# Rescheduling a fused attention and channel-mixing kernel: first scaling on VectorE, batch steps in other slots, four splits moved to the next pair

## The chip, the cores and the metric

One core of a Trainium2 chip runs the whole program. The metric is the device time in microseconds (us) of one execution, as the median of several.

## The reference, cut to what matters

For 8 batches of 576 tokens, 8 heads of 64, the reference packs k and v through 32 pack rows p, attends from q to the packed rows, and feeds the result through two channel-mixing layers.

```python
def _attn_ref(q, k, v, p):
    p_packed = sm_attn(p, k, v)            # softmax(p k^T / 8) v
    out = sm_attn(q, p_packed, p_packed)   # 576 tokens against 32 packed rows
def _moe_ref(x, ...):                      # xk, xr: x mixed with the token before it
    k = np.maximum(xk @ w_k, 0.0)          # 512 -> 1024
    v = k * k @ w_v                        # 1024 -> 512
    r = 1.0 / (1.0 + np.exp(-(xr @ w_r)))
    return r * v
def _moe2_ref(x, U, V, w_ch1, w_ch2):
    u = x + (x.transpose(0, 2, 1) @ U @ V).transpose(0, 2, 1)
    return u + np.maximum(u @ w_ch1, 0.0) @ w_ch2   # 512 -> 2048 -> 512
```

All is float32. Large products are made from a high and a low part of each operand in three passes of TensorE. The last two products (w_ch1, w_ch2) are made with 7 block products instead of 8, from sums of blocks.

## The kernel before, in words

**One order for all engines.** `everything` (L1263) walks one list of items; each engine's block runs its own share of each item, in that order, and semaphores do the rest. An item's place is thus its place in all engines' queues at once. DMAs are issued by SP (HWDGE), by ScalarE in the first loads, and by GpSimd (the first p and v, the constants, the weights of the first layer, and the pieces).

**Start** (`first_items`, L179). Batch 0's attention runs alone, in the order of `UNIT_STEPS`: kA, kB (VectorE transposes k's four column blocks, L634/L636), p (GpSimd scales p by 1/8, L1477; VectorE transposes it, L648), scores1 (L532), a (L540), qA, pv (L552), pp (L558), qB, scores2 (L566), two softmax halves (sm, then norm0 and norm1, L677 to L688), outA and outB (L579). After scores2 and outB, TensorE makes 88 and 32 idle transposes (L1551). GpSimd issues p's four DMAs, v's ten, then scales p, then issues the constants (mu, U), then the weights' chunks, of which it also makes the low parts (L1507).

**Stage A** (`chunk_plan`, L121). Four groups of two batches (1152 tokens), each in 3 chunks of 384 tokens; the groups are called FIRST, MIDDLE (twice) and LAST. A chunk has 17 slots: 8 of k (12 matmuls of 384 columns, L780), 3 of r (12 of 512, L759), 6 of v (12 of 512, L794). Slots are counted through a group, 0 to 50. `batch_plans` (L98) puts the steps of the batches to come into slots: in group g a "second" batch (2g+1), a "third" (2g+2), and a "fourth" (2g+3), whose steps from slot 51 on fall into the next group ("rest"). A step is run behind the slot's own work. ("mix", "split") make a chunk's inputs from the attention's output x (L719, L732, L744, L751). `pe_g` (L863) reduces x2 with U. ScalarE and VectorE square k and split it (L814, L837, L803, L830).

**Pieces.** 32 pieces of w_ch1 and w_ch2 are loaded, combined by GpSimd (L1238 to L1243), split by ScalarE and VectorE (L1255, L1260) and stored in DRAM for stage B. The first `EARLY` of them use one buffer, during FIRST and MIDDLE, at the slots of `FIRST_AT` and `EARLY_AT`; the others (`piece_items`, L208) run in LAST with four buffers.

**Stage B** (`pair_plan`, L254). Five pairs of token tiles (512 wide three times, then 384), each with two groups g of hidden blocks; per g a first product m1 (4 units i of 7 positions, L1035) and a second m2 (28 entries e, L1121), each entry six matmuls with weights from `w_ring`, which SP loads 11 entries ahead (L1365). A pair's input u (L935, L940) is made during the pair before, its sums by GpSimd (L961 to L973), and its 14 combinations are split by ScalarE and VectorE (L994, L1000) as ("us", p, k). Position pos of m1 needs k = 2 pos and 2 pos + 1. In a pair's first unit `pe_m1` writes into banks that stage A has just used (`trio`, L456).

Of the kernel before, what the change touches and what calls it, by code (L numbers as in the profile page):

```python
# [34 lines left out]
VLOADS = 10  # L35
# [36 lines left out]
EARLY, FIRST_AT, EARLY_AT = 20, (22, 29, 36, 44), (0, 5, 10, 15, 23, 29, 35, 40)  # L72
# [25 lines left out]
def batch_plans(kind):  # L98


    third = (2, batch_slots(15, 17, 19, 20, 21, 22, 23, 25, 26, 28, 31, 33, 35))
    fourth = batch_slots(37, 39, 41, 42, 43, 44, 45, 47, 48, 50, 53, 55, 58)
    here = (3, {at: steps for at, steps in fourth.items() if at < CHUNKS * NSLOT})
    rest = (1, {at - CHUNKS * NSLOT: steps for at, steps in fourth.items() if at >= CHUNKS * NSLOT})
    if kind == FIRST:
        second = {2: ("scores1",), 4: ("a",), 5: ("qA",), 6: ("pv",), 7: ("qB", "pp"), 8: ("scores2",), 9: ("sm1",),
                  10: ("norm0",), 11: ("norm1",), 13: ("outA",), 14: ("outB",)}
        return [(1, second), third, here]
    return [rest, third, here] if kind == MIDDLE else [rest]
# [13 lines left out]
def chunk_plan(c, kind):  # L123
# [6 lines left out]
    for at, slot in enumerate(SLOTS):  # L130
# [32 lines left out]
        if kind == FIRST and c == 0 and at in (5, 6):  # L163
            items.append(("mix" if at == 5 else "split", 1, 0))
# [42 lines left out]
def piece_items():  # L207


    plan = {9: [("ws_load", EARLY + m) for m in range(SLOTS_P + 1)]}  # L210
    for m in range(PIECES - EARLY):
        n, at = EARLY + m, 12 + 8 * m // 5
# [36 lines left out]
U_SPOTS = [(0, 1), (0, 4), (1, 1), (1, 4), (2, 5), (3, 1), (3, 3), (3, 5)]  # L249
TURN_AT = (5, 11, 17, 23)  # L250


def pair_plan(p, left, turns):
# [3 lines left out]
    for g in range(NG):  # L257
        for i in range(NU):
            for pos in range(NPROD):
                items.append(("m1", g, i, pos))  # L260
                if p == 0 and g == 0 and i == 0 and pos < 5:
                    items += [[("x2s", 7, PAIRS - 1)], [("g", 7, 1, PAIRS - 1)], [("x2s", 8, PAIRS - 1)],
                              [("g", 8, 1, PAIRS - 1)], [("g_evac", 1, PAIRS - 1)]][pos]
# [19 lines left out]
        for e in range(NPROD * NU):  # L283
# [21 lines left out]
            if g == NG - 1 and p < NB - 1 and e % 2 == 1:  # L305
                items.append(("us", p + 1, e // 2))
# [28 lines left out]
class Attention:  # L335


    def __init__(self, sb, sem, scope):
# [22 lines left out]
        self.v_first_in, self.v_in = sem("v_first_in"), sem("v_in")  # L361
# [14 lines left out]
def build(nc, q, k, v, p, mu_k, mu_r, w_k, w_v, w_r, u, vv, w1, w2, out):  # L376
# [79 lines left out]
    trio = [{"X": (2, 4), "Y": (4, 2), "Z": (3, 3)}, {"X": (7, 5), "Y": (5, 7), "Z": (6, 6)}]  # L456
# [64 lines left out]
    def pe_attn(pe, n, step):  # L521
# [21 lines left out]
        elif step == "pv":  # L543
            if isinstance(n, int) and n == 0:
                pe.wait_ge(L.v_first_in, VLOADS * 16)
            else:
                pe.wait_ge(L.v_in, VLOADS * 16 * n)
# [92 lines left out]
    def dve_attn(dve, n, slot, step, mixes):  # L640
# [5 lines left out]
        elif step == "p":  # L646
            dve.wait_ge(L.p_scaled, n + 1)
# [355 lines left out]
    def pe_m1(pe, p, g, i, pos):  # L1003
# [7 lines left out]
        if pos in (R11, T1) and i < 2:  # L1011
# [3 lines left out]
            elif (pos, i) == (R11, 1):  # L1015
                pe.wait_ge(g_hi, B)
                pe.wait_ge(g_lo, B)
            elif (pos, i) == (T1, 1):
                pe.wait_ge(x2_ok, TPC * (NCH + 1))
# [722 lines left out]
```

## Time and profile before

| | us |
|---|---|
| median of 3 runs | 1409.76 |
| lowest, highest | 1403.69, 1412.27 |
| profiled execution | 1406.93 |
| its span, first to last instruction | 1405.1 |
| TensorE busy in the span | 1326.8 (94%) |
| VectorE, ScalarE, GpSimd busy | 912.5, 726.4, 222.5 |

TensorE is busy nearly all the time, so a time is read here as TensorE's work plus TensorE's idle stretches. Mean granted clock of TensorE is 0.988 of full. The start, up to TensorE's first matmul, takes 22.2 us; stage A ends at about 656 us; stage B and the last stores fill the rest.

### The profile page before, as it was taken

To read this page: it belongs to the slowest core of one execution; us is meant where nothing else is said; L and a number is where in the kernel's file an instruction comes from. 1 tells how busy PE (TensorE), PEld (TensorE's weight loads), DVE (VectorE), ACT (ScalarE), POOL (GpSimd) and SP (SyncE) were. 2 spreads that over 40 slices of the span, in tenths; PEclk is the share of its full clock that TensorE was granted. 3 is DMA by queue.
4 is the path that set the end of the run, shared out by engine and by line. 5 is a ranking of instruction groups with operands and counts; after the bars stand their busy time and mean duration, and the time that the engine had idled before them with its cause. 6 is when DMAs were issued, how large, how long until landed. Compare 5 with 4: busy or idle time off the path is not lost.

```text
span 1405.1 us, 21457 instructions
## 1 busy us (share of the span) xinstructions
PE 1326.8 (94%) x7712; PEld 1137.3 (81%) x7712; DVE 912.5 (65%) x1489; ACT 726.4 (52%) x1274; POOL 222.5 (16%) x306
## 2 busy tenths in 40 slices
PE   2889999999999999999999999999999999899997
PEld 1767787887888788987888788887888898899996
DVE  2777777677766876844563766549473776466746
ACT  1565664575557556644544645455453644365543
POOL 5830112212131103502000300012000200020000
PEclk9989999999999999999999999999999999999999
DMA  9653454555536512953756578765887578878986
GB/s 173 165 107 71 140 105 137 145 121 143 139 106 148 138 55 71 297 186 125 235 191 211 165 223 233 211 208 177 236 220 220 179 229 230 261 239 253 269 267 158
DMA packets 377001, 252.52 MB, mean 180 GB/s; under 512 B 249120, under 2 KB 291200, under 8 KB 376896
## 3 DMA queue, kind: packets, MB, share of 16 engines
q1 hardware_dynamic: 367136, 238.66, 60.3%
q0 software_dynamic: 5024, 11.90, 2.8%
q8 instruction: 62, 1.02, 0.3%
q10 hardware_dynamic: 4736, 0.59, 0.3%
q14 instruction: 43, 0.35, 0.1%
HBM read 201.25 MB, written 49.81 MB: 179 GB/s over the span
## 4 chain that ended last, share of the span: by engine, by line
PE 75%; DVE 10%; DMA 4%; issue 3%; ACT 3%; SPq 2%; POOL 2%; DVEq 0%; ACTq 0%; POOLq 0%
PE bank L1035 24%; PE bank L1121 21%; PE bank L780 9%; PE bank L794 9%; PE bank L759 6%; SPq L1295 2%; DMA w_ring<-w_parts 2%; PE bank L935 1%; DVE mixed L732 1%; DVE hid_parts L1150 1%; PE bank L863 1%; PE bank L579 1%; DVE acc L1169 1%; DMA early_raw<-in_moe_w_ch 1%; DVE u_parts L1000 1%
## 5 line engine op out<-in xcount | busy, mean ns | idle before, releaser
L1121 PE MATMUL bank<-hid_parts,w_ring 128*128 128x512 f32 (+1 forms) x1680 | 356.5, 370 | 10.0 <-DMA w_ring<-w_parts 4.7
L1035 PE MATMUL bank<-u_parts,w_ring 128*128 128x512 f32 (+1 forms) x1680 | 354.8, 369 | 2.8 <-ACT hid L1057 2.8
L1121 PEld LDWEIGHTS bank<-hid_parts,w_ring 128*128 128x128 f32 x1680 | 302.9, 188 | 62.1 <-issue 16.2
L1035 PEld LDWEIGHTS bank<-u_parts,w_ring 128*128 128x128 f32 x1680 | 306.2, 188 | 41.4 <-issue 3.1
L1144 ACT ACTIVATE hid_parts<-hid_raw 128x512 fp32r<-128x512 f32 (+1 forms) x280 | 164.8, 589 | 145.3 <-PE bank L1121 143.9
L1150 DVE TENSOR_TENSOR hid_parts<-hid_raw,hid_parts 128x512 fp32r<-128x512 f32 (+1 forms) x280 | 185.8, 669 | 67.0 <-ACT hid_parts L1144 63.4
L780 PE MATMUL bank<-xk_hi,wk_hi 128*128 128x384 f32 x384 | 132.1, 344 | 3.5 <-DVE xk_lo L751 3.5
L780 PE MATMUL bank<-xk_lo,wk_hi 128*128 128x384 f32 x384 | 130.0, 338 | 0.0
L780 PE MATMUL bank<-xk_hi,wk_lo 128*128 128x384 f32 x384 | 129.9, 338 | 0.0
L1080 DVE TENSOR_TENSOR hid_raw<-bank,hid_z 128x512 f32<-128x512 f32 (+1 forms) x40 | 25.5, 638 | 154.4 <-PE bank L1035 154.3
L794 PE MATMUL bank<-wv_hi,k_hi 128*128 128x512 f32 x288 | 113.4, 394 | 0.0
L794 PE MATMUL bank<-wv_lo,k_hi 128*128 128x512 f32 x288 | 112.2, 390 | 0.0
L794 PE MATMUL bank<-wv_hi,k_lo 128*128 128x512 f32 x288 | 112.1, 389 | 0.0
L814 ACT ACTIVATE square<-bank 128x384 f32<-128x384 f32 x96 | 47.0, 490 | 121.6 <-PE bank L780 101.3
L837 DVE TENSOR_TENSOR square<-square 128x384 f32<-128x384 f32 x96 | 57.3, 598 | 66.9 <-ACT square L814 66.5
L961 POOL TENSOR_TENSOR u_sums<-acc 128x512 f32<-128x512 f32 (+1 forms) x10 | 11.8, 1180 | 509.9 <-ACT acc L950 509.9
L780 PEld LDWEIGHTS bank<-xk_hi,wk_hi 128*128 128x128 f32 x384 | 73.3, 191 | 11.3 <-issue 8.6
L732 DVE SCALAR_TENSOR_TENSOR mixed<-x,mu,mixed 128x384 f32<-128x384 f32 x96 | 58.0, 666 | 32.1 <-ACT mixed L719 32.1
L1169 DVE TENSOR_TENSOR acc<-bank,acc 128x512 f32<-128x512 f32 (+1 forms) x120 | 73.9, 630 | 7.6 <-PE bank L1121 7.5
L780 PEld LDWEIGHTS bank<-xk_lo,wk_hi 128*128 128x128 f32 x384 | 73.3, 191 | 1.4
L780 PEld LDWEIGHTS bank<-xk_hi,wk_lo 128*128 128x128 f32 x384 | 73.1, 190 | 0.0
L794 PEld LDWEIGHTS bank<-wv_hi,k_hi 128*128 128x128 f32 x288 | 54.0, 188 | 13.8 <-issue 2.3
(156 smaller groups left out, 1934.5 us busy)
## 6 DMA issues: line engine op xcount, KB each, us to landing
w_ring<-w_parts SPq DMA_DIRECT2D x560, 256.0 KB, 3.5
w_parts<-early_out SPq DMA_DIRECT2D x23, 896.0 KB, 4.9
x_scratch<-x SPq DMA_DIRECT2D x36, 256.0 KB, 2.1
kq_parts<-in_k SPq DMA_DIRECT2D x120, 72.0 KB, 2.7
kq_parts<-in_q SPq DMA_DIRECT2D x112, 72.0 KB, 2.3
w_parts<-piece_out SPq DMA_DIRECT2D x9, 896.0 KB, 6.0
v_rows<-in_v SPq DMA_DIRECT2D x56, 128.0 KB
out_dram<-acc SPq DMA_DIRECT2D x84, 64.0 KB, 3.4
```

The lines of the kernel that those rows point to most:

```text
L732: last = nc.vector.scalar_tensor_tensor(out3, segments(c, ft, 0), mu[:, which, ft:ft + 1], out3, ALU.mult, ALU.add)
L759: last = nc.tensor.matmul(bank, a, b_, start=(done == 0), stop=(done == 3 * n_terms - 1))
L780: last = nc.tensor.matmul(bank[:, 0:CHUNK], wk[a][:, ct, at * P:(at + 1) * P], xk[b_][:, ct, :], start=(ct == 0 and a == 0 and b_ == 0), s ...
L794: last = nc.tensor.matmul(bank, k2[a][:, f, at * P:(at + 1) * P], wv[b_][:, f, :], start=(f == 0 and a == 0 and b_ == 0), stop=(f == NFA - ...
L814: nc.scalar.activation(square[:, at % 2, :], bank[:, 0:CHUNK], ACT.Relu).then_inc(k_ev, 1)
L837: nc.vector.tensor_tensor(square[:, at % 2, :], square[:, at % 2, :], square[:, at % 2, :], ALU.mult).then_inc(squared, 1)
L1035: last = nc.tensor.matmul(to, wring[:, e % RW, ct, a, :], uc[:, pos, b, ct, 0:w], start=(pos in FRESH and ct == 0 and a == 0 and b == 0), ...
L1121: last = nc.tensor.matmul(role(st, j, BANK_OF[pos])[:, 0:w], wring[:, e % RW, j, a, :], hid[:, no % RH, b, 0:w], start=(pos in FRESH and i ...
L1144: nc.scalar.activation(hid[:, no % RH, 0, 0:w], raw[:, pos, i, 0:w], ACT.Copy).then_inc(hid_hi, 1)
L1150: nc.vector.tensor_tensor(hid[:, no % RH, 1, 0:w], raw[:, pos, i, 0:w], hid[:, no % RH, 0, 0:w].bitcast(F32), ALU.subtract).then_inc(hid_l ...
L1169: nc.vector.tensor_tensor(to, role(st, j, name)[:, 0:w], to, ALU.add).then_inc(sum_ok, 1)
L1295: eng.dma_start(part[32 * quad:32 * quad + 32, :, :], src).then_inc(done, 16)
```

## The change

1. **First p and v.** VectorE waits for the first p's DMAs and scales it itself, in front of its transpose. GpSimd issues 6 of v's 10 first DMAs; ScalarE's queue issues the other 4, behind its part of k. TensorE's pv waits for both.
2. **Slots.** Steps of the third and fourth batch get other slots, in MIDDLE far earlier ones and more evenly spread (third from slot 6 instead of 15, fourth from 32 instead of 37). The second batch's steps move by up to one slot in FIRST; the first chunk's second mix and split move from slots 5 and 6 to 3 and 5.
3. **Pieces.** 18 instead of 20 run early, at other slots; the 14 of LAST begin three slots earlier.
4. **Stage B.** Per pair, 10 of the 14 splits stay in the m2 of the pair before, at 10 of its 28 entries; k = 10 to 13 move to the first four positions of the pair's own first unit. Before stage B's second unit, the last g work of stage A is spread over seven positions instead of five, with the banks of Z and X swapped on side 1 so that its bank is needed later.

```diff
-EARLY, FIRST_AT, EARLY_AT = 20, (22, 29, 36, 44), (0, 5, 10, 15, 23, 29, 35, 40)
+EARLY, FIRST_AT, EARLY_AT = 18, (23, 31, 38, 45), (0, 6, 11, 17, 23, 33, 40)
@@ batch_plans
-    third = (2, batch_slots(15, 17, 19, 20, 21, 22, 23, 25, 26, 28, 31, 33, 35))
-    fourth = batch_slots(37, 39, 41, 42, 43, 44, 45, 47, 48, 50, 53, 55, 58)
+    if kind == FIRST:
+        third = batch_slots(15, 17, 19, 20, 21, 22, 23, 25, 26, 28, 30, 34, 36)
+        fourth = batch_slots(37, 38, 40, 41, 42, 43, 44, 45, 47, 49, 50, 53, 55)
+    else:
+        third = batch_slots(6, 8, 11, 13, 15, 16, 17, 19, 21, 23, 25, 28, 30)
+        fourth = batch_slots(32, 33, 35, 37, 38, 39, 40, 42, 45, 47, 50, 53, 55)
-        second = {2: ("scores1",), 4: ("a",), 5: ("qA",), 6: ("pv",), 7: ("qB", "pp"), 8: ("scores2",), 9: ("sm1",),
-                  10: ("norm0",), 11: ("norm1",), 13: ("outA",), 14: ("outB",)}
+        second = {2: ("scores1",), 4: ("a",), 6: ("pv", "qA"), 7: ("qB",), 8: ("pp",), 9: ("scores2",),
+                  10: ("sm1", "norm0"), 11: ("norm1",), 13: ("outA",), 14: ("outB",)}
@@ chunk_plan
-        if kind == FIRST and c == 0 and at in (5, 6):
-            items.append(("mix" if at == 5 else "split", 1, 0))
+        if kind == FIRST and c == 0 and at in (3, 5):
+            items.append(("mix" if at == 3 else "split", 1, 0))
@@ piece_items
-    plan = {9: [("ws_load", EARLY + m) for m in range(SLOTS_P + 1)]}
+    plan = {6: [("ws_load", EARLY + m) for m in range(SLOTS_P + 1)]}
-        n, at = EARLY + m, 12 + 8 * m // 5
+        n, at = EARLY + m, 9 + 8 * m // 5
@@ pair_plan
+US_AT = (1, 4, 7, 9, 12, 15, 18, 20, 23, 25)
-                if p == 0 and g == 0 and i == 0 and pos < 5:
-                    items += [[("x2s", 7, PAIRS - 1)], [("g", 7, 1, PAIRS - 1)], [("x2s", 8, PAIRS - 1)],
-                              [("g", 8, 1, PAIRS - 1)], [("g_evac", 1, PAIRS - 1)]][pos]
+                if p == 0 and g == 0 and i == 0:
+                    items += {0: [("x2s", 7, PAIRS - 1)], 2: [("g", 7, 1, PAIRS - 1)], 3: [("x2s", 8, PAIRS - 1)],
+                              5: [("g", 8, 1, PAIRS - 1)], 6: [("g_evac", 1, PAIRS - 1)]}.get(pos, [])
+                if p > 0 and g == 0 and i == 0 and pos < 2 * NPROD - len(US_AT):
+                    items.append(("us", p, len(US_AT) + pos))
-            if g == NG - 1 and p < NB - 1 and e % 2 == 1:
-                items.append(("us", p + 1, e // 2))
+            if g == NG - 1 and p < NB - 1 and e in US_AT:
+                items.append(("us", p + 1, US_AT.index(e)))
@@ build
-    trio = [{"X": (2, 4), "Y": (4, 2), "Z": (3, 3)}, {"X": (7, 5), "Y": (5, 7), "Z": (6, 6)}]
+    trio = [{"X": (2, 4), "Y": (4, 2), "Z": (3, 3)}, {"X": (6, 5), "Y": (5, 6), "Z": (7, 7)}]
@@ pe_attn, dve_attn
-                pe.wait_ge(L.v_first_in, VLOADS * 16)
+                pe.wait_ge(L.v_first_in[0], 16 * 6)
+                pe.wait_ge(L.v_first_in[1], 16 * (VLOADS - 6))
+            if isinstance(n, int) and n == 0:
+                dve.wait_ge(L.p_first_in, 64)
+                nc.vector.tensor_scalar(L.pz[:, :, :], L.pz[:, :, :], SCALE, None, ALU.mult).then_inc(L.p_scaled, 1)
@@ pe_m1: the waits of (R11, unit 1) and (T1, unit 1) change places
@@ gpsimd
-        load_v(pool, 0)
-        scale_p(0)
+        load_v(pool, 0, range(6), att.v_first_in[0])
-                if k == 4:
+                if k == 2:
                     scale_p(2 * g + 3)
@@ scalar, start_loads
+                load_v(act, 0, range(6, VLOADS), att.v_first_in[1])
```

## Rows read from the trace of the kernel before

**Rows 1.** The page, parts 1 and 2: engines' busy time; granted clock in slices

```profile
PE 1326.8 (94%) x7712; PEld 1137.3 (81%) x7712; DVE 912.5 (65%) x1489; ACT 726.4 (52%) x1274; POOL 222.5 (16%) x306
PEclk9989999999999999999999999999999999999999
```

**Rows 2.** Waits of TensorE, 60 to 640 us: total us, times, longest

```profile
PE bank L579 <- DVE kqT L688: 10.7, 4, 3.1
PE bank L558 <- DVE packed L661: 4.9, 1, 4.9
PE bank L540 <- ACT probs L590: 1.6, 3, 0.8
PE bank L759 <- DVE xr_lo L751: 1.4, 1, 1.4
```

**Rows 3.** Timeline of the start: start, duration, engine, line [idle before]

```profile
5.36 4.79 POOL L1310 DMA_DIRECT2D v_rows<-in_v  x7
...
14.32 0.67 DVE L634 STREAM_TRANSPOSE kqT<-kq_parts 128x512 f32<-128x512 f32 x1
...
19.13 0.68 POOL L1310 DMA_DIRECT2D v_rows<-in_v  x1 [8.99 <-issue]
...
21.03 0.57 POOL L1477 TENSOR_SCALAR p_parts<-p_parts 128x128 f32<-128x128 f32 x1
...
21.64 0.31 DVE L648 STREAM_TRANSPOSE pT<-p_parts 128x128 f32<-128x128 f32 x1 [6.52 <-POOL p_parts L1477]
```

**Rows 4.** Tile views, p_parts then kq_parts_early, 0 to 60 us: DMA landing

```profile
DMA to landing us min/median/max: 2.7/3.0/3.5
DMA to landing us min/median/max: 2.9/6.1/10.4
```

**Rows 5.** Timeline, batch 0's last q blocks and what waits for them

```profile
6.55 18.30 SPq L1295 DMA_DIRECT2D kq_parts_early<-in_q  x16
...
30.85 1.43 DVE L638 STREAM_TRANSPOSE kqT<-kq_parts_early 128x576 f32<-128x576 f32 x2
...
32.43 1.20 PE L566 MATMUL bank<-kqT,packedT 64*32 64x288 f32 x32 [1.18 <-DVE kqT L638]
```

**Rows 6.** Windows: length, busy PE, PEld, DVE, ACT, POOL, PEclk, DMA share, GB/s

```profile
12.00:20.00 8.00, 0.00 (x0) 0.00 (x0) 2.27 (x6) 0.00 (x0) 0.87 (x2) 1.00 1.23 134
81.10:91.20 10.10, 6.46 (x29) 4.32 (x37) 7.81 (x15) 5.14 (x9) 3.42 (x6) 0.50 0.57 120
169.80:173.20 3.40, 3.40 (x24) 2.25 (x13) 2.71 (x4) 0.65 (x1) 1.03 (x3) 0.50 0.66 241
```

**Rows 7.** Timeline, the first chunk and the mix before it

```profile
49.93 5.17 DVE L732 SCALAR_TENSOR_TENSOR mixed<-x,mu,mixed 128x384 f32<-128x384 f32 x4 [1.39 <-ACT mixed L719]
...
79.60 2.19 DVE L732 SCALAR_TENSOR_TENSOR mixed<-x,mu,mixed 128x384 f32<-128x384 f32 x4
```

**Rows 8.** Lines of VectorE, 269.7 to 294.3 us

```profile
L830 DVE TENSOR_TENSOR k_lo<-square,k_hi 128x384 fp32r<-128x384 f32 x8 | 4.7, 583 | 0.0
```

**Rows 9.** Windows: a MIDDLE group's second chunk, its k slots

```profile
269.70:291.50 21.80, 21.80 (x225) 19.84 (x224) 15.60 (x31) 11.87 (x24) 4.72 (x8) 1.00 0.75 152
```

**Rows 10.** Waits of TensorE, 660 to 1165 us

```profile
PE bank L863 <- DVE x2s_lo L874: 1.6, 1, 1.6
```

**Rows 11.** Windows: end of the first pair, around entries 20 to 24

```profile
800.00:806.00 6.00, 5.37 (x22) 3.85 (x22) 6.00 (x9) 3.25 (x6) 2.48 (x2) 1.00 0.46 154
```

**Rows 12.** Waits of TensorE, 1165 to 1216 us

```profile
PE bank L1121 <- DMA w_ring<-w_parts: 4.7, 6, 1.8
PE bank L1035 <- ACT hid L1057: 2.8, 1, 2.8
```

**Rows 13.** Timeline of VectorE, one k_lo of the first chunk

```profile
71.85 1.09 DVE L830 TENSOR_TENSOR k_lo<-square,k_hi 128x384 fp32r<-128x384 f32 x1
```

**Rows 14.** Lines of VectorE, 309 to 320 us: two of norm0's and norm1's five operations

```profile
L688 DVE STREAM_TRANSPOSE kqT<-probs 128x576 f32<-128x576 f32 x2 | 1.6, 780 | 0.1
...
L677 DVE TENSOR_REDUCE tok_sum<-probs 128x18 f32<-128x576 f32 x2 | 1.5, 744 | 0.0
```

## What is predicted, and from what

> **What bounds the kernel now.** I read the page first: TensorE is busy 1326.8 of 1405.1 us and its clock is near full in every slice but the third [rows 1]. VectorE is far behind with 65%. So the change can win only TensorE's 78.3 us of idleness, and the half-clock stretches that follow some of it. Of the 78.3, 22.2 lie before the first matmul and the stores behind the last one also count; I looked for the rest in TensorE's waits. In stage A they are few and large: outA (L579) waits four times for the last transpose of a batch's normalised scores (10.7 us together, longest 3.1), pp waits once 4.9, the first r product once 1.4 [rows 2]. Stage B waits for little until 1165 us [rows 10, 11]; behind that lie 4.7 us for the weight ring and 2.8 for an evacuation held up by output stores [rows 12]. The last two are transfers' waits and no edit touches them; I count nothing there.
>
> The windows add the clock: 0.50 from 81.1 to 91.2 and from 169.8 to 173.2 [rows 6], and the same 3.4 us long from 320.0, where the third wait ends. Each begins during or right behind one of the waits of [rows 2] (1.2 for 2.4 GHz). At half clock the busy TensorE time does half its work: 6.46 / 2 = 3.2 us lost in the first, 3.4 / 2 = 1.7 in each of the others.
>
> **The start.** p's DMAs are issued in front of v's, which begin at 5.36 [rows 3], and land at most 3.5 us after their issue [rows 4], so p is there by about 9. GpSimd issues seven of v's DMAs, then stands 8.99 us, issues the rest and scales p at 21.03; VectorE, done with k at about 15.1, idles 6.52 us for it [rows 3]. After the change VectorE scales at 15.1. No row has this operation on VectorE; the bounds are 0.1 and GpSimd's 0.57, and I take the transpose of the same tile, 0.31. scores1 then starts near 15.9 instead of 22.2, 6.2 us earlier. What is late next is q: its last issue ends at 24.85, it lands 2.9 to 10.4 us after issue [rows 4, 5], and VectorE's last two q transposes took it without a wait at 30.85 [rows 5]. So it landed between 27.3 and 30.85; scores2 needs it plus 1.43 and ran at 32.43. With the middle, 29.1, scores2 comes at 30.7: gain 1.7. If only the second transpose is left after a landing at 27.3 it is 28.2, gain 4.2. On the other side, the weights' loads wait for VectorE's qA and now start some 5 us earlier, among q's last DMAs; a q that takes its longest landing, 10.4 after 24.4, gives scores2 at 36.3, a loss of 3.9. I take 1.7, range -3.9 to +4.2. Four DMAs on ScalarE's queue cost it nothing: its first work was the exponential behind scores1. Splitting v I count at nothing: the DMA share is 1.23 from 12 to 20 us [rows 6], so a second queue adds no transfer rate, and pv did not wait for v.
>
> The Trainium skill has the rule that speaks against this part (DMA: Bandwidth & Descriptors, "Issuing engines are not separate DMA queues": transfers from different engines share the same 16 DMA engines, a second issuer saves issue time only). By it the split of v brings 0; if a second queue were a second path, q would come early and the start would gain the whole 6.2. The share over 1 agrees with the rule.
>
> **The first chunk.** TensorE stands 4.9 us for pp, 1.4 for xr_lo, and loses 3.2 to the clock: 9.5 at stake. Now the mix comes two slots earlier and pp stands behind the first r. But a mix in slot 3 costs ScalarE 2.1 and VectorE 2.2 to 5.2 us in front of the copies that pv needs. Against TensorE's order, with 2.2, pv waits some 2 us and the first r starts at about 81 instead of 85.2; with 5.2 xr_lo is ready at 83. So 2.2 to 4.2 of the 6.3 idle, and the clock's 3.2 perhaps: range 2 to 9.5. I take 3.2 and half of the clock's, 4.8.
>
> The two prices of the mix are a row each: 5.17 us for four operations at 49.93, beside GpSimd's weight splits, and 2.19 at 79.60, when those end [rows 7]. The Trainium skill has a rule that speaks against this edit (SBUF — State Buffer, "Who interferes with whom": a VectorE instruction with two SBUF inputs contends with a GpSimd one that reads SBUF). Slot 3 lies among GpSimd's splits, so by the rule the edit brings 2.2, by the later row 4.2 plus the clock; the trace agrees with the rule at 49.93.
>
> **FIRST and MIDDLE.** In FIRST, outA waits 3.1 (slot 33) and 2.9 (slot 55), in each MIDDLE group once (slot 33; 2.2 and 2.7): the 10.7 of [rows 2]. All four have one cause: norm1, about 2.7 us of VectorE (five operations, three of some 0.75 [rows 14] and two small), stands two slots ahead of outA and behind a mix, a split or a piece. After the change the distance is four and three slots in FIRST, three in MIDDLE (8 us of TensorE). I count all 10.7, and the two clock stretches, 3.4: 14.1. Bounds: 0, if norm1 is late all the same, and 14.1. Steps that only spread cost no more work. In a MIDDLE group's second chunk the k slots get two softmax halves (three operations of 0.75 each) and norm0 (2.7), 7.2 us by the sizes of [rows 14], for transposes and maxima of about 6.9: VectorE goes from 15.6 of 21.8 [rows 9] to some 16 of about 19.3, since scores1, a and pv leave these slots. Busier, not full, but steps now arrive just in time at places where there was room. Such near misses are in the trace, L540's: three of 0.5 us [rows 2]. I take ten new ones at that price off, 5 us; bounds 0 and 10.
>
> **Pieces, loads.** Two pieces go from the early group to LAST, which starts three slots (7.6 us) earlier at the same rate; SP's loads wait only for batch 7's outB, now at slot 4 instead of 7. Cover: TensorE's own work in LAST, which had no idle stretch. Without cover one piece's 1.4 MB at 300 GB/s is 4.7 us, 9.4 in all. Scaling p for a fourth batch now stands in front of piece 3 instead of 5, long after its load. Nothing.
>
> **Stage B.** The g product in the first unit waits 1.6 us for VectorE, busy with splits [rows 10]; one position (1.37) later: 1.3, between 0 and 1.6. At the first pair's end VectorE is busy 6.00 of 6.00 us while TensorE idles 0.63 [rows 11]; four splits fewer are 4 x 0.68 = 2.7 us less of VectorE there. With the stretch before it and three more pairs' ends, 4 x 0.7 or 2.8 are at stake (an estimate from this one); I take 2.0, between 0 and 2.8. The four moved splits stand in front of left-over sums, 0.68 each, in a unit where VectorE has slack.
>
> **Sum.** 1.7 + 4.8 + 14.1 + 1.3 + 2.0 = 23.9, less 5: 18.9 us. Against the profiled span 1405.1 that is 1386.2. That execution took 1406.93; the median of the runs is 2.8 above it, so the median should go from 1409.8 to 1390.9.
>
> **Rivals.**
> - *The waits move along.* VectorE works in order; what was late at outA is late at pp, xr_lo or scores2. Then half of 23.9 comes and the 5 us of new waits stay: about 7, so 1403. For it: VectorE's share rises in the k slots. Against it: all four outA waits had one pattern.
> - *The first 90 us give nothing.* The weights' loads push q back (-3.9) and the first mix costs 5.2 (2.2): 18.9 - 5.6 - 2.6 = 10.7, so 1399. For it: the share over 1 [rows 6] and the 5.17 of [rows 7].
> - *Slower: VectorE overruns in the k slots.* If its 16 squares and low parts of a chunk run at 1.09 [rows 13] instead of 0.58 [rows 8] because of GpSimd, VectorE needs 16.0 + 16 x 0.51 = 24.2 for 19.3 us of TensorE: 4.9 lost in each of six chunks, 29, against 24 won and with the 5 of new waits: +10, so 1420. It decides once the mean passes 0.9. Against it: GpSimd is busy only 4.72 of 21.8 us there [rows 9], and has fewer pieces.
> - *Nothing happens.* It would need every moved step to be hidden; with waits of 22.2 and 10.7 that go by name I give it no chance of its own beside the first rival.
>
> **Chances.** The sum 0.62, on its own 1383 to 1396; waits moving along 0.25; first 90 us 0.08; slower 0.05. The range 1382 to 1403 takes in the first three down to the moving waits. A measurement tells about 1%, 14 us, from no change: below 1395.7 is faster. The forecast's case gives faster 0.62, the next two the same 0.33, the last slower 0.05.
>
> **What the profile would show.** scores1 at 16 and scores2 near 31; no wait over 1 us at L579 and L558; clock 1.00 at 170 and 320; first r near 82; g at stage B's start within 0.5 us; VectorE under 6 of 6 at the pairs' ends; and the waits of [rows 12] as they are. I am wrong if L558, L540 or L566 gather waits of 2 us in FIRST and MIDDLE, or if the stretch behind 1165 grows.

## The result, and the profile after

The changed kernel takes 1396.8 us (median of 6 executions, 1391.45 to 1400.04) against 1408.5 for the kernel before (6 executions beside it): ratio 0.9911, 95% interval 0.9882 to 0.9941. That is 12.5 us less (0.0089 x 1408.5). It lies inside the predicted range of 1382 to 1403 and 5.9 above the predicted 1390.9; it is just outside the 1383 to 1396 that the prediction gave its sum on its own, and above the 1395.7 below which it called the change faster. Three executions of kernels of the experiments (1486.5, 2671.7 and 3002.2 us) lie far above all others of the same kernel and are in no ratio. The profiled execution has a span of 1390.6 us, 14.5 less than before.

The page of the changed kernel, parts 1 and 2 (to be laid beside [rows 1]):

```profile
PE 1326.0 (95%) x7712; PEld 1136.3 (82%) x7712; DVE 912.7 (66%) x1490; ACT 717.4 (52%) x1268; POOL 214.1 (15%) x297
PEclk9899999999999999999999999999999999999998
```

TensorE's busy time hardly moves (1326.8 to 1326.0), as it should: its idle time falls from 78.3 to 64.6. Its waits from 60 to 640 us (engine, line and releaser: us in total, times, longest; L770, L547 and L874 are r, "a" and g), against [rows 2]:

```profile
PE bank L770 <- DVE xr_lo L762: 3.5, 1, 3.5
PE bank L770 <- ACT square L825: 2.2, 2, 1.8
PE bank L874 <- DVE x2s_lo L885: 1.9, 2, 1.4
PE bank L547 <- ACT probs L598: 1.3, 2, 0.7
PE bank L946 <- DVE v L1703: 1.2, 1, 1.2
```

All four outA waits (10.7 us in [rows 2]) are gone, and so is pp's of 4.9. The first r's wait for xr_lo grew from 1.4 to 3.5. r's wait for ScalarE's square is new, and g's for x2s_lo grew from 0.5 (before's row below) to 1.9.

```profile
PE bank L863 <- DVE x2s_lo L874: 0.5, 1, 0.5
```

Timeline of the start (start, duration, engine, line, in brackets the idle time before and its releaser), against [rows 3, 5]:

```profile
14.85 0.71 DVE L642 STREAM_TRANSPOSE kqT<-kq_parts 128x512 f32<-128x512 f32 x1 [7.37 <-DMA kq_parts<-in_k]
...
17.05 0.19 DVE L657 TENSOR_SCALAR p_parts<-p_parts 128x128 f32<-128x128 f32 x1
...
17.84 2.17 PE L539 MATMUL bank<-kqT,pT 64*32 64x288 f32 x32 [17.84 <-DVE pT L659]
...
25.99 1.60 POOL L1501 DMA_DIRECT2D stage_r<-in_moe_w_k  x3 [3.16 <-DVE kqT L646]
...
26.32 0.33 PE L566 MATMUL bank<-ident,packed 128*128 128x128 f32 x1 [0.57 <-DVE packed L672]
...
31.32 0.78 DVE L646 STREAM_TRANSPOSE kqT<-kq_parts_early 128x576 f32<-128x576 f32 x1 [3.12 <-DMA kq_parts_early<-in_q]
...
32.24 2.18 PE L574 MATMUL bank<-kqT,packedT 64*32 64x288 f32 x32 [5.59 <-DVE kqT L646]
```

scores1 comes 4.4 us earlier, pp 4.6, and scores2 0.2: a wait of 5.6 us for q has taken nearly the whole gain. Windows of the changed kernel (length, busy PE, PEld, DVE, ACT, POOL, PEclk, DMA share, GB/s): the start, the first r, the places of the two half-clock stretches of [rows 6], and the first pair's end [rows 11]:

```profile
28.00:38.30 10.30, 6.06 (x51) 4.72 (x52) 4.66 (x7) 1.39 (x2) 0.82 (x2) 0.50 0.97 291
82.60:89.50 6.90, 5.87 (x14) 4.57 (x15) 6.80 (x14) 3.09 (x5) 1.75 (x3) 0.51 0.43 132
168.50:172.00 3.50, 3.50 (x22) 3.50 (x22) 3.50 (x7) 1.61 (x4) 1.44 (x2) 1.00 0.55 182
317.00:321.00 4.00, 4.00 (x49) 3.11 (x48) 4.00 (x7) 2.82 (x5) 1.76 (x3) 1.00 0.89 150
787.50:793.50 6.00, 5.91 (x26) 4.28 (x25) 5.95 (x9) 3.08 (x6) 1.77 (x2) 1.00 0.56 168
```

The two stretches in stage A are at 1.00. The one of the first chunk is 6.9 us long instead of 10.1, and there is a new one of 10.3 us at the start, where before ran at full clock:

```profile
28.00:38.30 10.30, 8.63 (x159) 7.39 (x158) 6.14 (x11) 2.83 (x5) 2.84 (x6) 1.00 1.00 302
```

Added up from the first matmul to 1300 us, the profile before has 27.3 us at half clock and the changed one has 27.3 as well: what stage A won back, the start took.

Stage B's waits, against [rows 10, 12] (L1046 is m1, L1132 m2):

```profile
PE bank L1046 <- DVE hid_raw L1091: 0.9, 1, 0.9
...
PE bank L1132 <- DMA w_ring<-w_parts: 3.2, 4, 1.1
PE bank L1046 <- ACT hid L1068: 2.4, 1, 2.4
```

To see where time comes from, take the moment at which TensorE starts a stage and compare it with the same moment in the profile of before. In us, negative is earlier (the kernels of the last columns follow below):

| TensorE starts | before at | changed | without part 1 | slots alone | chunk alone | part 4 alone | start alone |
|---|---|---|---|---|---|---|---|
| scores2, batch 0 | 32.43 | -0.2 | +0.5 | -0.2 | -1.0 | +0.5 | +6.4 |
| first k | 56.12 | +0.7 | +0.5 | -0.7 | -1.0 | -0.2 | +6.7 |
| first r | 85.21 | -1.6 | -2.1 | 0.0 | -3.6 | +0.3 | +7.8 |
| k, FIRST's second chunk | 116.19 | -1.5 | -2.4 | -1.2 | -4.0 | -0.8 | +6.6 |
| k, second MIDDLE, first chunk | 372.94 | -10.6 | -10.9 | -11.8 | -2.4 | -1.9 | +4.2 |
| k, LAST's first chunk | 518.99 | -11.7 | -11.9 | -15.3 | +1.5 | -1.9 | +5.5 |
| stage B | 656.7 | -12.2 | -13.5 | -17.2 | -0.3 | -3.7 | +3.7 |
| second pair's m1 | 821.45 | -13.4 | -14.6 | -17.2 | -0.4 | -4.9 | +3.7 |
| third pair's m1 | 983.03 | -14.3 | -15.6 | -17.2 | -0.4 | -5.8 | +3.7 |
| fifth pair's m1 | 1276.46 | -15.6 | -17.2 | -13.9 | +1.4 | -5.8 | +1.6 |

One profile is one execution, and executions of one kernel lie up to 9 us apart (23 of the kernel before run from 1401.7 to 1410.7); a column shows where steps come, not their size to the microsecond.

### The profile page after: what moved, and what is told of

Read it like the earlier page. It is cut to its first block, busy times and chain, and to the rows that moved or that the text cites. A ratio compares the mean times of both kernels' runs of the same rounds, so it can differ in the third digit from the quotient of the medians.

```text
span 1390.6 us, 21451 instructions
## 1 busy us (share of the span) xinstructions
PE 1326.0 (95%) x7712; PEld 1136.3 (82%) x7712; DVE 912.7 (66%) x1490; ACT 717.4 (52%) x1268; POOL 214.1 (15%) x297
## 4 chain that ended last, share of the span: by engine, by line
PE 76%; DVE 9%; SPq 6%; DMA 4%; issue 2%; ACT 2%; POOL 0%; DVEq 0%; ACTq 0%
PE bank L1046 25%; PE bank L1132 23%; PE bank L805 9%; PE bank L791 8%; PE bank L770 6%; SPq L1306 3%; DVE mixed L743 2%; DMA w_ring<-w_parts 1%; PE bank L946 1%; SPq L1321 1%; DMA w_parts<-early_out 1%; PE bank L1559 1%; PE bank L874 1%; PE bank L587 1%; DVE square L848 1%
## 5 line engine op out<-in xcount | busy, mean ns | idle before, releaser
L1132 PE MATMUL bank<-hid_parts,w_ring 128*128 128x512 f32 (+1 forms) x1680 | 356.4, 370 | 6.6 <-DMA w_ring<-w_parts 3.2
L1046 PE MATMUL bank<-u_parts,w_ring 128*128 128x512 f32 (+1 forms) x1680 | 355.4, 369 | 3.8 <-ACT hid L1068 2.4
L1132 PEld LDWEIGHTS bank<-hid_parts,w_ring 128*128 128x128 f32 x1680 | 302.9, 188 | 58.5 <-issue 14.1
L1046 PEld LDWEIGHTS bank<-u_parts,w_ring 128*128 128x128 f32 x1680 | 305.8, 188 | 43.5 <-issue 4.4
L972 POOL TENSOR_TENSOR u_sums<-acc 128x512 f32<-128x512 f32 (+1 forms) x10 | 11.7, 1179 | 493.4 <-ACT acc L961 493.4
L791 PEld LDWEIGHTS bank<-xk_hi,wk_hi 128*128 128x128 f32 x384 | 72.9, 190 | 14.9 <-issue 9.4
L743 DVE SCALAR_TENSOR_TENSOR mixed<-x,mu,mixed 128x384 f32<-128x384 f32 x96 | 59.9, 684 | 29.1 <-ACT mixed L730 28.8
L805 PEld LDWEIGHTS bank<-wv_hi,k_hi 128*128 128x128 f32 x288 | 54.0, 188 | 15.9 <-issue 4.0
```

The lines of the kernel that those rows point to most:

```text
L743: last = nc.vector.scalar_tensor_tensor(out3, segments(c, ft, 0), mu[:, which, ft:ft + 1], out3, ALU.mult, ALU.add)
L791: last = nc.tensor.matmul(bank[:, 0:CHUNK], wk[a][:, ct, at * P:(at + 1) * P], xk[b_][:, ct, :], start=(ct == 0 and a == 0 and b_ == 0), s ...
L805: last = nc.tensor.matmul(bank, k2[a][:, f, at * P:(at + 1) * P], wv[b_][:, f, :], start=(f == 0 and a == 0 and b_ == 0), stop=(f == NFA - ...
L1046: last = nc.tensor.matmul(to, wring[:, e % RW, ct, a, :], uc[:, pos, b, ct, 0:w], start=(pos in FRESH and ct == 0 and a == 0 and b == 0), ...
L1132: last = nc.tensor.matmul(role(st, j, BANK_OF[pos])[:, 0:w], wring[:, e % RW, j, a, :], hid[:, no % RH, b, 0:w], start=(pos in FRESH and i ...
```

## Experiments: each part alone

**Part 1 alone** (the first p and v as in the changed kernel, all else as before):

```
+            if isinstance(n, int) and n == 0:
+                dve.wait_ge(L.p_first_in, 64)
+                nc.vector.tensor_scalar(L.pz[:, :, :], L.pz[:, :, :], SCALE, None, ALU.mult)...
-        load_v(pool, 0)
-        scale_p(0)
+        load_v(pool, 0, range(6), att.v_first_in[0])
+                load_v(act, 0, range(6, VLOADS), att.v_first_in[1])
```

> The kernel before with part 1 of the change alone (VectorE scales the first p, v over two queues). Two theories. Clock theory: q still lands last, near 31, so scores2 stays at 32.2; TensorE idles 5.6 us in front of it and drops to half clock there, so the 88 idle transposes end late, outA comes at about 46.0 instead of 44.9, the first k group at 56.8 instead of 56.1 and batch 1's scores1 at 65.7 instead of 64.1: +1.5 us in all, ratio 1.000 to 1.002. Rival, as the prediction had it: the 4.4 us that scores1 gains are partly kept, first k group at 54.4 or sooner and 1.7 us off the total, ratio 0.9988.

1410.1 us against 1406.3, ratio 1.0027 [1.0008, 1.0047], 12 executions: 3.8 us slower. Its timeline:

```profile
37.85 0.78 DVE L639 STREAM_TRANSPOSE kqT<-kq_parts_early 128x576 f32<-128x576 f32 x1 [8.89 <-DMA kq_parts_early<-in_q]
...
38.78 2.18 PE L567 MATMUL bank<-kqT,packedT 64*32 64x288 f32 x32 [12.18 <-DVE kqT L639]
```

The last block of q is there at 37.8, beyond even the prediction's worst case (a scores2 at 36.3). Of the two theories on record neither had this; the one that expected a loss had q near 31 and 1.5 us.

**The changed kernel without part 1** (the lines above undone).

> The changed kernel without part 1. Clock theory: the first r group comes at 82.0 instead of 83.6 and everything behind it 1.6 us earlier, total 1395.2 against 1396.8, ratio 0.990. Rival (the start did help): first k group as before at 56.1 but total 1 to 4 us above the changed kernel, ratio 0.992 to 0.994.

1388.9 us, 0.9878 [0.9858, 0.9898]. That is 4.6 us better than the changed kernel (0.0033 of 1406), and its 4 executions lie within 4.3 us, the changed kernel's within 8.6. Both numbers that were expected (0.990, or 0.992 to 0.994) were too high. The two intervals overlap a little (0.9882 to 0.9898), so the size is uncertain, but with everything else in place part 1 seems to cost as much as alone. Its profile has 17.1 us at half clock up to 1300 us, where the changed kernel's has 27.3.

**Third and fourth batch's slots alone.** `EARLY`, the pieces' slots, the second batch and stage B are as before; the MIDDLE groups' lines of the edit:

```
-    third = (2, batch_slots(15, 17, 19, 20, 21, 22, 23, 25, 26, 28, 31, 33, 35))
-    fourth = batch_slots(37, 39, 41, 42, 43, 44, 45, 47, 48, 50, 53, 55, 58)
+        third = batch_slots(6, 8, 11, 13, 15, 16, 17, 19, 21, 23, 25, 28, 30)
+        fourth = batch_slots(32, 33, 35, 37, 38, 39, 40, 42, 45, 47, 50, 53, 55)
```

> The kernel before with the third and fourth batches' slots alone (pieces, first chunk, start and stage B as before). If the waits of outA are removed by the slots themselves: no wait over 1 us at L579 behind 100 us, full clock at 170 and 320 us, and about 10 us off (4.9 in FIRST, 5.3 in MIDDLE as the changed kernel shows them), ratio 0.993. Rival: the slots need the new places of the pieces (18 instead of 20 early ones, six slots apart) and without them ScalarE or VectorE holds up the k groups; then 3 to 6 us off, ratio 0.996 to 0.998.

1392.9 us, 0.9905 [0.9887, 0.9922]: 13.4 us, where about 10 was expected; the rival, that the slots need the pieces' new places, fell. The table's column goes from -1.2 to -15.3 by LAST: 14.1. Its waits from 60 to 640 us still have those of the first chunk, and at outA's matmuls none for kqT (one of 0.4 for x):

```profile
PE bank L562 <- DVE packed L665: 4.5, 1, 4.5
PE bank L536 <- DVE pT L652: 2.0, 2, 1.1
PE bank L763 <- DVE xr_lo L755: 1.4, 1, 1.4
```

**Part 4 alone.** In short:

```
+US_AT = (1, 4, 7, 9, 12, 15, 18, 20, 23, 25)
-            if g == NG - 1 and p < NB - 1 and e % 2 == 1:
+            if g == NG - 1 and p < NB - 1 and e in US_AT:
```

> The kernel before with part 4 alone (four splits into the next pair, g work spread, banks swapped). From the changed kernel's trace: 0.2 us at stage B's start, 1.0 us at the end of each of pairs 1, 2 and 4, and at most 0.9 in the ring's waits behind 1165 us: 3.4 off, less 1.1 that the last stores took back, ratio 0.998. Rival: the gain of pairs 3 and 4 in the changed kernel was the DMA's chance and not the splits'; then only the first two pairs' ends gain, 2.0, ratio 0.9985, and the waits for the ring stay at 4.7.

1403.7 us, 0.9983 [0.9969, 0.9997]: 2.4 us. The column's -3.7 at the start of stage B is no effect of it, as stage A is that of before: 1.8 of it is u's wait of 1.7 at 619 us, which before's profile has and this one hasn't. Its own are the two steps of 1.0 at the first and second pair's ends.

**The first chunk alone** (with the second batch's slots):

```
-        if kind == FIRST and c == 0 and at in (5, 6):
+        if kind == FIRST and c == 0 and at in (3, 5):
```

> The kernel before with the first chunk's edit alone: the second batch's steps in their new slots of FIRST, and the first chunk's second mix and split in slots 3 and 5. Theory: what the whole changed kernel gained between the first k and the first r product (2.3 us; 2.6 without part 1) belongs to this edit alone, and the next outA too: first r 2.5 us earlier than before, the end 2.5 to 5 us earlier, ratio about 0.9975. Rival: the edit gains nothing alone (the waits at L579 behind it are met again later): ratio 1.000. By the prediction's term of 4.8 it would be 0.9966.

1401.7 us, 0.998 [0.9966, 0.9994]: 2.8 us. First r is 3.6 earlier, 2.6 of it behind the first k. In this profile the gain is lost again, and the waits from 60 to 640 us and the windows say how:

```profile
PE bank L579 <- DVE kqT L688: 12.2, 4, 4.1
PE bank L759 <- DVE xr_lo L751: 4.0, 1, 4.0
```

```profile
233.00:237.00 4.00, 4.00 (x15) 3.65 (x15) 2.23 (x4) 1.94 (x5) 2.10 (x4) 0.57 0.05 19
465.50:472.30 6.80, 5.50 (x29) 4.33 (x30) 4.19 (x6) 0.65 (x1) 1.74 (x4) 0.50 0.58 196
```

The same places in the kernel before:

```profile
233.00:237.00 4.00, 1.11 (x19) 0.36 (x18) 3.86 (x8) 1.42 (x3) 1.20 (x2) 1.00 0.82 260
466.00:470.00 4.00, 2.19 (x24) 1.61 (x25) 3.93 (x7) 0.65 (x1) 0.00 (x0) 1.00 0.93 309
```

In this execution two of the four outA waits became longer (3.2 for 2.9 and 4.1 for 2.7), and the clock fell behind both, which before's profile passed at full clock. But it took 1408.4 and is the slowest of its twelve: by time, over all twelve, the 2.8 us do arrive.

## Experiments: why the start costs

**Weights' loads held back.** The changed kernel, with the loads of the first layer's weights waiting for all eight transposes of k and q.

```
-        pool.wait_ge(att.kq_ok, CT + 2)
+        pool.wait_ge(att.kq_ok, KQ)
```

> The changed kernel, but GpSimd starts the weights' loads only when all of batch 0's q is transposed (a wait for 8 instead of 6). Rival theory (the weights' 2.6 MB among q's last DMAs push q back): q lands near 29, scores2 at 30 or below, first k group not before 55.5, total 3 to 5 us below the changed kernel, 1392 to 1394. If v's second queue is what counts: q lands near 30.5 to 31, scores2 at 31.5 to 32, and the weights, 4 us later, hold up the first k group or the first v group instead; total the same or 1 to 3 us more, 1397 to 1400.

1388.5 us, 0.9887 [0.9867, 0.9906]; timeline:

```profile
29.43 0.78 DVE L646 STREAM_TRANSPOSE kqT<-kq_parts_early 128x576 f32<-128x576 f32 x1 [1.30 <-DMA kq_parts_early<-in_q]
30.36 2.17 PE L574 MATMUL bank<-kqT,packedT 64*32 64x288 f32 x32 [4.29 <-DVE kqT L646]
30.51 1.60 POOL L1501 DMA_DIRECT2D stage_r<-in_moe_w_k  x3 [7.11 <-DVE kqT L646]
```

The weights start at 30.5 instead of 26.0, q is in at 29.4 instead of 31.3, scores2 gains 2.1 over before, and weights that come later held nothing up: the first k is 1.7 and the first r 4.0 us earlier than before. The time came out 4 us better than the 1392 to 1394 expected, though the ratio's interval and the changed kernel's still overlap (0.9882 to 0.9906).

**The same edit on part 1 alone.**

> The kernel before with part 1 of the change alone, and GpSimd's loads of the first weights waiting until VectorE has transposed all eight column blocks of q and k (instead of the first six). Theory: part 1 by itself cost 6.4 us at scores2 because the weights' loads, asked for 5 us earlier, ran among q's last DMAs; with the wait q is in by about 29.5, scores2 comes near 30.4 to 30.9 (32.43 before), the first r product not later than before, and the ratio is at or below 1.000 (about -1.5 us, 0.999). Rival: it is v's split over two queues that pushes q back (k's last block already landed 2 us later with it); then q still lands behind 31, scores2 comes at 33 or later and the ratio stays near 1.0027. Second rival: weights that come late hold up the first chunk by 2 us or more, then scores2 is early and the first k product is not.

```profile
29.08 0.78 DVE L639 STREAM_TRANSPOSE kqT<-kq_parts_early 128x576 f32<-128x576 f32 x1 [0.82 <-DMA kq_parts_early<-in_q]
...
30.01 2.18 PE L567 MATMUL bank<-kqT,packedT 64*32 64x288 f32 x32 [3.36 <-DVE kqT L639]
```

q is in at 29.1 instead of 37.8, with v still on two queues. All six profiles that have part 1 with the split agree: with the weights' loads beside, q's last block is in at 31.2, 31.3 and 37.8, with the weights held back at 28.8, 29.1 and 29.4. So the weights' loads are needed for the delay. Whether they are enough is for the next experiment. First r is 1.9 earlier than before, FIRST's last r 3.4. By time it is 1.0009 [0.9993, 1.0025]: no longer a loss that shows, but no gain either (and the interval overlaps that of part 1 alone). In its profile 3.4 at 193 us is 1.5 at 244 and a loss of 2.2 at 489. It meets the same outA waits as the first chunk alone does (3.3 at 233 us and 3.1 at 467 with a half-clock stretch behind each). The expectation had the place right and the end wrong.

**All of v on GpSimd's queue** (otherwise the changed kernel).

> The changed kernel, all ten first loads of v on GpSimd's queue again, VectorE still scaling the first p. Theory (v on ScalarE's queue takes DMA time from k and q on SP's): k lands near 13 instead of 14.8, scores1 near 15.5 to 16, q lands near 29.5 instead of 31.3, scores2 near 30.5, the idle stretch in front of it under 4 us; total 3 to 5 us below the changed kernel, 1392 to 1394, ratio 0.989. Rival (the weights' loads alone push q back): q still lands at 31 or later and the total stays within 1 us of the changed kernel's, ratio 0.991.

1396.0 us, 0.9940 [0.9921, 0.9959], not better than the changed kernel. Of q, though, the theory was right and the rival wrong: the weights' loads start even earlier, at 25.1, and the last two blocks of q are transposed from 29.98 without a wait for their loads.

```profile
25.06 1.61 POOL L1500 DMA_DIRECT2D stage_r<-in_moe_w_k  x3
29.98 1.43 DVE L645 STREAM_TRANSPOSE kqT<-kq_parts_early 128x576 f32<-128x576 f32 x2
31.56 2.17 PE L573 MATMUL bank<-kqT,packedT 64*32 64x288 f32 x32 [2.12 <-DVE kqT L645]
```

So it seems to take both, the weights' loads and the split, to make q late; either remedy brings it in by 30 (this one in a single profile). What the split does shows on SP's queue: its sixteen issues of q end at 25.7 to 27.4 us in the six profiles with the split, and at 24.7 here (24.4 to 26.3 in the seven without part 1). Its waits from 20 to 80 us:

```profile
PE bank L547 <- ACT probs L597: 6.1, 2, 4.3
PE bank L790 <- POOL wk_lo L1514: 4.3, 1, 4.3
PE bank L559 <- DMA v_rows<-in_v: 3.4, 1, 3.4
```

pv now waits 3.4 for v, which the prediction had left out. Its first k also waits for GpSimd's low part of the weights (4.3), and batch 1's "a" waits 4.3; that those come from the single queue isn't shown. "The split counts at nothing" was thus wrong twice: it makes q's issue later, and it covers a wait of 3.4. By time the theory that one queue would be better fell. scores1 comes 1.4 earlier than in the changed kernel, but that is no effect of the queue: VectorE takes k's last three blocks from 12.4 to 14.9 us in the six profiles with the split and from 12.4 to 14.1 in the eight without, one as scattered as the other.

**40 idle transposes behind the first pp,** to keep the clock up over the wait for q.

```
-IDLE_TURNS = {(0, "scores2"): 88, (0, "outB"): 32}
+IDLE_TURNS = {(0, "pp"): 40, (0, "scores2"): 88, (0, "outB"): 32}
```

> The changed kernel with 40 more idle transposes of TensorE between pp and scores2 (4.4 us at full clock), in the stretch in which it waits for q. Clock theory: the clock stays at 1.00 from 28 to 38, scores2 takes 1.2 us, the 88 idle transposes end in front of outA, outA comes at 45.0 instead of 46.0 and the first k group near 55.8; 1 to 2 us off, ratio 0.990. Rival (the clock after 28 us does not matter, VectorE's chain of norm0 and norm1 sets outA): outA stays at 46.0 and the total at the changed kernel's, ratio 0.991.

In the profile it does what it should: no half clock until 54.8 us, scores2 in 1.21 us, first r 3.4 earlier than before, a span of 1383.1. But that is the fastest of the 11 executions compared, which run from 1385.4 to 1404.3, and the ratio is 0.9959 [0.9937, 0.9980]: the 0.990 expected was missed, and by time the edit gains nothing over the changed kernel. Clock explains a third of that scatter: the spans 1383.1 and 1401.7 have mean clocks of 0.994 and 0.990, a loss of 0.006 x 1383 = 8.3 against 0.010 x 1402 = 14.0 us. The rest stays open; the weights' loads are not held back in it, and its longer executions left no trace.

## Experiments: what the pieces cost

The column "slots alone" is 3.6 us ahead of the changed kernel at LAST. **The changed kernel without parts 1 and 3:**

```
-EARLY, FIRST_AT, EARLY_AT = 18, (23, 31, 38, 45), (0, 6, 11, 17, 23, 33, 40)
+EARLY, FIRST_AT, EARLY_AT = 20, (22, 29, 36, 44), (0, 5, 10, 15, 23, 29, 35, 40)
```

> The changed kernel without part 1 and without part 3: pieces as before (20 early ones at the old slots, LAST's from slot 9). Theory: in the changed kernel the piece of slot 17 is stored by SP only behind the ten loads of v that go out in slot 17, so ScalarE waits 4.8 us for the buffer at slot 23 and TensorE 1.8 us at the r group (437 us) and 0.4 to 1.3 in the group before; with the piece at slot 15 the store goes out first. Then no wait of TensorE for L825's counterpart at r, stage A ends some 3 us earlier and the total is 1386 (ratio 0.9857). Rival: the loss against slots_only lies in the two pieces more in LAST or in chance; then the total stays at 1389, ratio 0.988.

1387.9 us, 0.9878 [0.9863, 0.9894]: the same ratio as without part 1 alone, which is what the rival had expected. Its profile though is at -17.6 at LAST's first chunk and -19.5 at LAST's last r, where the version without part 1 has -11.9 and -13.5. The changed kernel's timeline shows a cause, SP's queue first:

```profile
418.54 7.61 SPq L1321 DMA_DIRECT2D v_rows<-in_v  x8
426.18 1.84 SPq L1325 DMA_DIRECT2D v_rows<-in_v  x2
428.07 11.43 SPq L1364 DMA_DIRECT2D w_parts<-early_out  x2
...
435.70 0.95 ACT L1266 ACTIVATE early_out<-early_raw 128x896 fp32r<-128x896 f32 x1 [4.82 <-DMA w_parts<-early_out]
...
437.08 0.50 PE L770 MATMUL bank<-wr_hi,xr_hi 128*128 128x512 f32 x1 [1.76 <-ACT square L825]
```

The piece of slot 17 is stored by SP, in order, behind ten v loads; ScalarE, which needs the one buffer, stands 4.8 us, its squares come late, and r waits for them. **One number changed** puts the store in front of the loads (on the version without part 1):

```
-EARLY_AT = (0, 6, 11, 17, 23, 33, 40)
+EARLY_AT = (0, 6, 11, 15, 23, 33, 40)
```

> The changed kernel without part 1, with one number changed: the MIDDLE groups' fourth piece is stored from slot 15, not 17, which puts its store in front of the ten v loads on SP's queue instead of behind them. Theory: those stores, held up to 428.07, were what kept ScalarE waiting 4.8 us for the piece buffer and TensorE 1.8 (and about 1 in the other MIDDLE group): both waits go, the profile's end of stage A comes 2 to 4 us earlier than without the edit, and the time is 1 to 3 us below 1388.9 (ratio 0.987 or less). Rival: the extra time of the new pieces' schedule comes from the work of two fewer early and two more late pieces, or from the other slots: then the end of stage A moves by under 1 us, and the ratio stays 0.9878.

```profile
415.42 1.39 SPq L1359 DMA_DIRECT2D w_parts<-early_out  x1
416.85 8.90 SPq L1317 DMA_DIRECT2D v_rows<-in_v  x8
...
429.06 0.95 ACT L1262 ACTIVATE early_out<-early_raw 128x896 fp32r<-128x896 f32 x1
```

ScalarE doesn't wait, r doesn't wait, and stage A ends 3.7 us earlier in the profile (-17.2 against -13.5 at LAST's last r). The wait of ScalarE, 3.6 to 5.7 us at this place, is in all five profiles with the store in slot 17 and in none of the four that have the new slots and the store in slot 15; TensorE's wait for square behind it is over 1.6 us in four of the five and 0.4 at most in the fifth. The median, 1387.1 against 1388.9, moves as expected, but the ratios 0.9882 [0.9856, 0.9909] and 0.9878 cannot tell the two apart: shown in the trace, not by the time. The old pieces' profile is another 2.2 us ahead at that place; where these come from stays open.

**Both remedies together:** the changed kernel with the old pieces' schedule and the weights' loads held back.

> The changed kernel with the pieces' schedule of before (part 3 undone) and the first weights' loads waiting for all eight transposes. Theory: the two costs that the runs so far found in the changed kernel, q among the weights' loads (about 4 in the profiles) and the store behind v's loads (about 3 to 4 by the end of stage A), are separate and add up; stage A ends 20 us or more earlier than in the kernel before. The stretch behind 1150 us, limited by DMA, gives some of it back, so the time lies at 1384 to 1388 (ratio 0.985 to 0.988). Rival: part 1 gains nothing even then, and it comes out at or above the 1387.9 of the version without part 1 and part 3, scattering more widely.

1383.9 us, 0.9850 [0.9828, 0.9872], better than the kernel before and the changed one, and as expected; stage A ends 21.2 us earlier than before. The four executions compared lie at 1382.8 to 1384.3, below the lowest (1386.95) of the version without parts 1 and 3, though the intervals of the two ratios just overlap. So part 1 seems to pay, by some 3 to 4 us, once the weights wait and the outA waits are gone. With the new pieces that isn't seen by time (0.9887 with part 1 and held weights, 0.9878 without part 1), so it isn't shown. Page, part 1:

```profile
PE 1322.4 (96%) x7712; PEld 1135.3 (82%) x7712; DVE 909.6 (66%) x1490; ACT 717.5 (52%) x1268; POOL 214.8 (16%) x301
```

## Why the prediction was right, and where not

| part | forecast us | alone, by time |
|---|---|---|
| start | 1.7 (-3.9 to 4.2) | -3.8 [-6.6, -1.1] |
| first chunk | 4.8 (2 to 9.5) | 2.8 [0.8, 4.8] |
| FIRST and MIDDLE | 14.1 (0 to 14.1) | 13.4 [11.0, 15.9] |
| A to B, stage B | 3.3 | 2.4 [0.4, 4.4] |
| new waits | -5 | the whole less the four: -2.3, give or take some 6 |
| whole | 18.9 | 12.5 [8.3, 16.6] |

The total came out right within its range. Where the 6.4 us to the forecast went shows in the changed kernel's own column: up to FIRST's second chunk it gained 1.5 where start and first chunk were to bring 1.7 + 4.8 = 6.5; from there to LAST 10.2, where 14.1 - 5 = 9.1 was forecast; behind it 3.9 to the fifth pair, where 3.3 was.

- **The start** is the step that failed. The prediction took the middle of q's landing, 29.1, and left "the weights' loads now start some 5 us earlier, among q's last DMAs" as the lower end. That end came: q at 31.3 in the changed kernel, 37.8 with part 1 alone. The 5 us themselves were too many: the weights' issue moved only from 27.54 to 25.99, as it waits for two transposes of q that now wait for their own loads; with the DMA engines at a share of 1 (28 to 38 us; 1.23 in [rows 6]) that was enough, but not by itself: SP's issue of q also ended 2.0 us later (26.87 for 24.85), which goes with v's split. The split, counted at nothing, had its part: in the one profile of part 1 without it q was in by 30 in spite of weights' loads at 25.1. Besides, the new wait in front of scores2 brought 10.3 us at half clock, which the prediction had not priced; idle transposes and outA therefore end 1.1 later than before. With the weights held back scores2 gains 2.1 to 2.7, close to the 1.7 forecast: the sum was that of a start without the contention. That 29.1 itself was met (28.8 to 29.4) is luck, as it was only the middle of two bounds. Without part 1 the forecast sum is 18.9 - 1.7 = 17.2, and the runs give 0.0122 x 1406 = 17.2; that they agree to the decimal is chance. By these point values nearly all of the miss (6.4) is the start's (1.7 + 4.6), but the 4.6 is the difference of two ratios whose intervals overlap. VectorE's scaling took 0.19 (bounds 0.1 and 0.57); scores1 came at 17.8, not 15.9, as k's last block came 2 us later in this execution; in the five other profiles with part 1 and the split scores1 came at 15.3 to 16.8. The rule of the Trainium skill (DMA: Bandwidth & Descriptors, "Issuing engines are not separate DMA queues") agrees with what happened: the prediction used it for v alone, and GpSimd's weights and v's four loads on ScalarE's queue delayed SP's q between them, which was in at 31.3 instead of by 30.
- **The first chunk:** the mechanism held, the size was near the lower end, 2.8. pp's wait went, but the first r now waits 3.5 for xr_lo and the clock still falls, for 6.9 instead of 10.1 us. The mix in slot 3 took 3.16 us and the split that ends the wait 2.43, in VectorE's timeline:

```profile
74.31 3.16 DVE L743 SCALAR_TENSOR_TENSOR mixed<-x,mu,mixed 128x384 f32<-128x384 f32 x4
...
81.05 2.43 DVE L762 TENSOR_TENSOR xr_lo<-mixed,xr_hi 128x768 fp32r<-128x768 f32 x2
```

  The mix lies between the 2.19 and 5.17 of [rows 7]. In GpSimd's timeline a group of its splits runs from 72.23 to 76.00 and the next from 77.90, so one runs beside part of it; that this is why it took 3.16 is an inference. Of the 6.2 us of idleness in front of the first r, 2.7 went, inside the forecast 2.2 to 4.2; it is the clock that gave back less than the 1.6 hoped for, as TensorE's busy time at half clock only fell from 6.46 to 5.87 us.
- **FIRST and MIDDLE:** right in cause and size. All four waits and both stretches went, also with the slots alone; 13.4 by time against 14.1. It shows in full only with the slots alone (14.1 in the profile); in the changed kernel 10.2 of it is left at LAST.
- **Pieces at nothing** was wrong as an argument. The cover was looked for in LAST; the cost lies in MIDDLE, where slot 17's store passes behind v's loads on SP's queue, a queue that a moved step was not followed into. r's 2.2 and g's 1.4 more than before make 3.6 of the 5 us set aside for new waits, but come under two names and not as ten near misses of 0.5: the 5 was near by luck.
- **A to B:** g's wait of 1.6 is gone, but m1 waits 0.9 for VectorE's hid_raw right behind it: 0.2 us (-12.2 to -12.4 by the end of that unit) in place of 1.3. **Pairs' ends:** 1.0 each for the first two, TensorE idle 0.09 instead of 0.63 us in the six us of [rows 11]; the forecast's 2.0 is met, though VectorE is as full as before (5.95 of 6).
- **The transfers' waits behind 1150 us** stay, as said. What was not said: they take back gains. The slots alone are at -17.3 at 1060 us and at -13.9 behind them, the old pieces at -21.6 and -20.9; the changed kernel lost nothing there (-14.3 and -15.6). Which execution loses there was not settled.
- **Rivals.** "The first 90 us give nothing" (1399) was the nearest in time, and half of it, q behind the weights, is what happened; at 0.08 it was rated too low, since the DMA share over 1 was there to be read. "The waits move along" didn't come true in the changed kernel, where outA waits nowhere; but the single profiles of part 1 with held weights and of the first chunk alone look like it, as the old outA waits there take back what was gained. VectorE didn't overrun: k_lo stayed at 0.55 us. The prediction's "decides once the mean passes 0.9" doesn't follow from its own figures, by which 16.0 + 16 x 0.21 = 19.3 is reached at 0.79.

## What to carry to other kernels

When a step in front is made faster, list what its earlier end releases, and ask on which DMA engines that lands: loads that were harmless behind q's last DMAs cost some 4 us among them, and one wait constant took the loss away. A moved step is to be followed into every queue that serves it; a store that slipped behind ten loads made the next user of its buffer wait 5 us. And look behind a gain for the next recurring wait: in two profiles with the old outA waits in place, 3.4 and 4.4 us gained by 193 us were gone at 489.

## What the runs showed of the hardware

- Whether the clock falls behind a wait is not read from the wait's length: in the kernel before it fell behind 2.2 us at 320 and stayed at 1.00 behind 2.88 at 236 and 2.65 at 468; in the chunk alone it fell behind 3.2 and 4.1 at the same two places. A stretch of 3.4 us at half clock with TensorE busy costs 1.7 us, one of 6.8 twice that, which is the size of the edits studied here. The profiles add up to 10.2 to 34.1 us at half clock by 1300 us, and part of what separates them is this.
- A load's landing under contention has a long tail: q's last blocks, whose issue ended at 26.9 to 27.4 us in each of these three kernels, were in at 29.1 us with the weights' loads held and at 31.3 or 37.8 with them beside. The last two have the same start, line for line.
- Four loads of v on ScalarE's queue went with SP's sixteen issues of q ending at 25.7 to 27.4 us (six profiles) instead of 24.7 (one, with part 1 but all of v on GpSimd's queue).
- The same store, two slots of work earlier or later, was issued at 415.4 or 427.8 (with and without the edit): SP issues in order, and ten loads of v stood in front.
